# Last h of the expert stage turned inside the down product before it, first half of w_out split ahead of the y gathers, and the first four column groups of product_a computed token tile by token tile

## The reference

```python
# 1. attention in hash buckets: 2 x 8 heads, 768 positions, width 64
mask = q_bucket[:, :, :, None] == k_bucket[:, :, None, :]
scores = np.where(mask, scale * q @ k.T, -1e9); x = softmax(scores) @ v
# 2. mixture of experts: 8 experts, the best two for each token
h = np.maximum(x[mask] @ w1[e], 0.0)                 # 512 -> 1024
out[mask] += top2_w[mask, k, None] * (h @ w2[e])     # 1024 -> 512
# 3. last stage, with a rational activation
h = x @ w_in                                         # 512 -> 2048
P = a[0] + a[1]*h + a[2]*h**2 + a[3]*h**3
Q = 1 + abs(b[0])*abs(h) + abs(b[1])*h**2
return (P / (Q + 1e-6)) @ w_out                      # 2048 -> 512
```

## Time and profile before

| what | value |
|---|---|
| runs | 984.72, 986.96, 989.23 us; median 986.96 us |
| the profiled execution's own time | 987.53 us |
| its span | 985.7 us |
| PE busy | 915.6 us, 93% of the span |
| mean granted TensorE clock | 0.971 |
| mixture stage: end of the last down product | 685.77 us |
| last stage: first matmul of product_a, first of product_b | 702.90 and 717.02 us |

### The profile page before, as it was taken

One profiled execution on the slowest core, in us unless ns is written; L12 is line 12 of the kernel. 1 busy time (PEld: TensorE's weight loads), 2 busy tenths in 40 slices (PEclk: granted clock), 3 DMA queues, 4 the chain that ended last, 5 costly groups with the idle time before them and its releaser, 6 DMA issues.

```text
span 985.7 us, 17793 instructions
## 1 busy us (share of the span) xinstructions
PE 915.6 (93%) x5505; PEld 789.2 (80%) x5506; DVE 584.6 (59%) x1232; ACT 495.8 (50%) x886; POOL 451.2 (46%) x361
## 2 busy tenths in 40 slices
PE   6899999999963999999999999997599999999998
PEld 5788888888852888888888888885489999999997
DVE  7689888899774222322222222221499877877775
ACT  3677787777640222222222222220377777777775
POOL 5633353335444536545644446500767554453222
PEclk9999999999985999999999999999699999999999
DMA  9963454253326768967868587813621100110000
GB/s 203 265 208 91 121 133 124 82 126 88 138 103 203 243 211 265 289 211 236 277 212 253 184 276 239 264 61 118 215 63 65 50 28 22 53 43 0 33 1 32
DMA packets 88148, 143.63 MB, mean 146 GB/s; under 512 B 15522, under 2 KB 47778, under 8 KB 87586
## 3 DMA queue, kind: packets, MB, share of 16 engines
q1 hardware_dynamic: 46450, 72.19, 24.8%
q0 software_dynamic: 19328, 54.53, 17.2%
q10 hardware_dynamic: 22320, 16.26, 5.6%
HBM read 123.30 MB, written 19.66 MB: 145 GB/s over the span
## 4 chain that ended last, share of the span: by engine, by line
PE 69%; DVE 12%; issue 5%; DMA 5%; POOL 3%; SPq 2%; ACT 2%; ACTq 0%; another core or an unknown queue 0%; DVEq 0%; POOLq 0%
PE ps_s L1107 18%; PE ps_o L1132 17%; PE ps_s L1175 13%; PE ps_t L1161 6%; DVE mx L1266 4%; PE ps_m L1161 3%; PE ps_s L1161 3%; PE ps_s L1118 3%; DMA q_in<-in_q 2%; PE ps_t L989 2%; PE ps_o L1002 1%; DVE tile_t L1243 1%; DVE qm L1256 1%; DMA k_in<-in_k 1%; SPq L433 1%
## 5 line engine op out<-in xcount | busy, mean ns | idle before, releaser
L555 POOL TENSOR_TENSOR w_r<-raw,w_r 128x1024 f32 (+1 forms) x72 | 171.4, 2398 | 109.9 <-DMA raw<-in_moe_w 47.9
L1107 PE MATMUL ps_s<-w_r,xT 128*128 x744 | 179.9, 398 | 17.0 <-DVE xT L1480 17.0
L1132 PE MATMUL ps_o<-w_r,hT 128*128 x744 | 175.6, 392 | 2.6 <-DVE hT L1484 2.6
L1107 PEld LDWEIGHTS ps_s<-w_r,xT 128*128 128x128 f32 x744 | 139.4, 191 | 45.3 <-issue 17.2
L1132 PEld LDWEIGHTS ps_o<-w_r,hT 128*128 128x128 f32 x744 | 140.7, 189 | 32.2 <-issue 2.8
L1175 PE MATMUL ps_s<-w_r,g_r 128*128 128x512 f32 x576 | 145.3, 397 | 4.4 <-DVE g_r L1566 4.4
L1490 DVE COPY y_sb<-ps_o 128x512 f32<-128x512 f32 x31 | 21.4, 691 | 211.6 <-PE ps_o L1132 211.6
L1175 PEld LDWEIGHTS ps_s<-w_r,g_r 128*128 128x128 f32 x576 | 107.5, 190 | 25.0 <-issue 4.3
L690 POOL TENSOR_TENSOR m<-q,g_r 128x384 f32<-128x384 f32 x64 | 66.0, 1031 | 113.9 <-DVE g_r L1554 113.7
L832 ACT ACTIVATE hT<-ps_s 128x1024 fp32r<-128x1024 f32 x31 | 31.8, 1026 | 160.2 <-DVE y_sb L1490 121.7
L749 ACT ACTIVATE prob<-ps_s,nb,sc 128x768 f32<-128x768 f32 x96 | 95.1, 991 | 20.2 <-DVE nb L1271 19.6
(11 more groups left out here) (240 smaller groups left out, 1480.5 us busy)
## 6 DMA issues: line engine op xcount, KB each, us to landing
w_r<-in_moe_w POOLq DMA_DIRECT2D x32, 1024.0 KB, 8.0
raw<-in_moe_w SPq DMA_DIRECT2D x56, 512.0 KB, 3.7
q_in<-in_q SPq DMA_DIRECT2D x56, 176.0 KB, 3.5
k_in<-in_k SPq DMA_DIRECT2D x56, 176.0 KB, 4.5
xg<-x_slots ACTq DMA_DIRECT2D x124, 64.0 KB, 3.4
y_slots<-y_sb ACTq DMA_DIRECT2D x31, 256.0 KB, 4.2
raw<-in_moe_w SPq DMA_DIRECT2D x16, 256.0 KB, 2.9
raw<-in_moe_w_in SPq DMA_DIRECT2D x8, 512.0 KB, 5.4
```

The costliest lines, as they stand in the source:

```text
L555: pool.tensor_tensor(of_chunk(buf, 1, n), raw[:, par, :], of_chunk(buf, 0, n).bitcast(F), ALU.subtract).then_inc(split_done, 1)
L1107: mm = pe.matmul(ps_s[0][:, o * 512:o * 512 + 512], xT[:, par, part, c * P:c * P + P], w_r[:, buf, wpart, col:col + 512], start=(c == 0 an ...
L1132: mm = pe.matmul(ps_o[:, :], hT[:, part, c * P:c * P + P], w_r[:, buf, wpart, col:col + DM], start=(c == 0 and part == 0 and wpart == 0), ...
```

## The change

Three things change.

1. In the mixture stage `down(29)` is cut in two halves of four chunks. `turn_h(30)` stands between the halves. The turned h of slot 30 gets a place of its own, `hT_last` (where xT was), and y of slot 30 a PSUM bank of its own, the lower half of ps_t, so that `down(30)` no longer waits for the copy of y 29. VectorE splits h 30 before it copies y 29.
2. GpSimd makes the low parts of w_out's chunks 0 to 3 behind the first cast and ahead of the wait for the stored y, no longer behind the gathers and the second cast.
3. The first four groups of `product_a` (f = 0 to 3) in the first block are computed by token tile: 12 matmuls of 128 columns for each group and tile (`first_part`) instead of 12 matmuls of 384 columns for each group. `a_ready` is raised when a group's third tile is done. ScalarE and VectorE alternate the two steps of the three tiles, and tiles 1 and 2 are turned in ps_s[0], not in ps_t.

```diff
-    x2_bank = [ps_o[:, :], ps_t[:, 0:512], ps_t[:, 512:1024]]
     ps_b = [ps_s[0][:, 0:512], ps_s[0][:, 512:1024], ps_s[1][:, 0:512]]
+    x2_bank = [ps_o[:, :], ps_b[0], ps_b[1]]
+    def hT_of(i):
+        return hT_last if last_slot(i) else hT
+    def y_bank(i):
+        return ps_t[:, 0:512] if last_slot(i) else ps_o[:, :]
...
@@ GpSimd
             cast_hi(1, wout_h[0], DM, 0)
+            split_some(E + 1, 1, range(CHUNKS // 2))
             pool.wait_ge(y_pos_ready, 1)
...
             cast_hi(1, wout_h[1], DM, CHUNKS // 2)
-            split_some(E + 1, 1, range(4))
@@ ScalarE
-            for j in range(TB):
+            def scale_first(j):
                 act.wait_ge(y_first_got[j][0], 16)
                 act.activation(ps_b[j], y_first[:, j, 0, :], ACT.Copy, scale=wts[:, 0, j:j + 1]).then_inc(y_scaled, 1)
...
+            scale_first(0)
+            for j in range(1, TB):
+                x2_first_high(j - 1)
+                scale_first(j)
+            x2_first_high(TB - 1)
@@ TensorE
-            def down(i):
+            def down(i, part=range(FC)):
...
-                    for part, wpart in ((0, 0), (0, 1), (1, 0)):
+                    for half, whalf in ((0, 0), (0, 1), (1, 0)):
...
                 up(i, par)
-                down(i - 1)
+                if last_slot(i):
+                    down(i - 1, range(0, FC // 2))
+                    turn_h(i)
+                    down(i - 1, range(FC // 2, FC))
+                else:
+                    down(i - 1)
             slots(pe, pe_slot)
-            turn_h(SLOTS - 1)
             down(SLOTS - 1)
...
-            for j in range(TB):
+            def first_part(f, j):
+                cols = slice(j * P, j * P + P)
+                for c in range(DC):
+                    for wpart, part in ((0, 0), (0, 1), (1, 0)):
+                        mm = pe.matmul(ps_a[f][:, cols], w_r[:, 0, wpart, c * FF2 + f * P:c * FF2 + f * P + P],
+                                       x2T[:, 0, part, c, cols], start=(c == 0 and wpart == 0 and part == 0),
+                                       stop=(c == DC - 1 and wpart == 1))
+                if j == TB - 1:
+                    mm.then_inc(a_ready, 1)
+            def first_turn(j):
                 pe.wait_ge(x2_ready, j + 1)
                 turn_x2(x2_first[:, j], x2_bank[j])
+            first_turn(0)
             pe.wait_ge(split_done, (E + 1) * CHUNKS)
+            pe.wait_ge(x2T_ready, 1)
+            first_part(0, 0)
+            first_turn(1)
+            for f in range(1, LAG + 1):
+                first_part(f, 0)
+            first_turn(2)
+            for j in range(1, TB):
+                pe.wait_ge(x2T_ready, j + 1)
+                for f in range(LAG + 1):
+                    first_part(f, j)
...
-                    if f < FC2:
+                    if f < FC2 and not (first and f <= LAG):
                         product_a(n, par, f)
@@ VectorE
-                copy_y(i - 1, (i - 1) // 2, 1 - par)
+                if not last_slot(i):
+                    copy_y(i - 1, (i - 1) // 2, 1 - par)
             slots(dve, dve_slot)
             split_h(SLOTS - 1)
+            copy_y(SLOTS - 2, (SLOTS - 2) // 2, (SLOTS - 2) % 2)
             copy_y(SLOTS - 1, (SLOTS - 1) // 2, (SLOTS - 1) % 2)
...
-            for j in range(TB):
+            combine(0)
+            for j in range(1, TB):
+                split_x2(0, 0, j - 1, x2_bank[j - 1])
                 combine(j)
-            for j in range(TB):
-                split_x2(0, 0, j, x2_bank[j])
+            split_x2(0, 0, TB - 1, x2_bank[TB - 1])
```

More of the change, by code:

```diff
@@ L142, in fused_kernel @@
     y_sb = at("y_sb", 188 * KB + 512, [P, 2, DM], F)
+    hT_last = at("hT_last", 148 * KB, [P, 2, FF], R)
     c = [168 * KB]
@@ L403, in fused_kernel, with last_slot @@
     ps_a = [ps_s[1][:, 512:512 + TOK], ps_m[:, 0:TOK], ps_t[:, 0:TOK], ps_t[:, 512:512 + TOK]]
-    x2_bank = [ps_o[:, :], ps_t[:, 0:512], ps_t[:, 512:1024]]
     ps_b = [ps_s[0][:, 0:512], ps_s[0][:, 512:1024], ps_s[1][:, 0:512]]
+    x2_bank = [ps_o[:, :], ps_b[0], ps_b[1]]
+    def last_slot(i):
+        return isinstance(i, int) and i == SLOTS - 1
+    def hT_of(i):
+        return hT_last if last_slot(i) else hT
+    def y_bank(i):
+        return ps_t[:, 0:512] if last_slot(i) else ps_o[:, :]
     with nc.Block() as block:
@@ L831, in hT_hi_out @@
                 act.wait_ge(h_turned, i + 1)
-                act.activation(hT[:, 0, :], ps_s[1][:], ACT.Copy).then_inc(hT_hi, 1)
+                act.activation(hT_of(i)[:, 0, :], ps_s[1][:], ACT.Copy).then_inc(hT_hi, 1)
             def relu(i):
@@ L870, in _, with x2_first_high @@
             act.wait_ge(one_eps_set, 1)
-            for j in range(TB):
+            def scale_first(j):
                 act.wait_ge(y_first_got[j][0], 16)
                 act.activation(ps_b[j], y_first[:, j, 0, :], ACT.Copy, scale=wts[:, 0, j:j + 1]).then_inc(y_scaled, 1)
-            for j in range(TB):
+            def x2_first_high(j):
                 act.wait_ge(x2_turned, j + 1)
@@ L1119, in turn_h @@
                 mm.then_inc(h_turned, 1)
-            def down(i):
+            def down(i, part=range(FC)):
                 e = expert_of(i)
                 buf = e % 2
[L1125 to L1129, removed]
-                    for part, wpart in ((0, 0), (0, 1), (1, 0)):
-                        col = WCOLS + c * DM
[L1132 to L1135, removed]
+                if part[0] == 0:
+                    pe.wait_ge(split_done, e * CHUNKS + CHUNKS)
+                    pe.wait_ge(hT_ready, i + 1)
+                    if not last_slot(i) and (not isinstance(i, int) or i > 0):
+                        pe.wait_ge(y_ready, i)
+                for c in part:
+                    for half, whalf in ((0, 0), (0, 1), (1, 0)):
+                        col = WCOLS + c * DM
+                        mm = pe.matmul(y_bank(i), hT_of(i)[:, half, c * P:c * P + P], w_r[:, buf, whalf, col:col + DM],
+                                       start=(c == 0 and half == 0 and whalf == 0),
+                                       stop=(c == FC - 1 and half == 1))
+                if part[-1] == FC - 1:
+                    mm.then_inc(slot_done, 1)
             up(0, 0)
@@ L1483, in split_h @@
                 dve.wait_ge(hT_hi, i + 1)
-                dve.tensor_tensor(hT[:, 1, :], ps_s[1][:], hT[:, 0, :].bitcast(F), ALU.subtract).then_inc(hT_ready, 1)
+                dve.tensor_tensor(hT_of(i)[:, 1, :], ps_s[1][:], hT_of(i)[:, 0, :].bitcast(F), ALU.subtract).then_inc(hT_ready, 1)
             def copy_y(i, n, par):
@@ L1489, in copy_y @@
                     dve.wait_ge(y_stored[par], n * 16)
-                dve.tensor_copy(y_sb[:, par, :], ps_o[:, :]).then_inc(y_ready, 1)
+                dve.tensor_copy(y_sb[:, par, :], y_bank(i)).then_inc(y_ready, 1)
             for i in range(2):
```

## The result

| | median us | runs | ratio to before, 95% interval |
|---|---|---|---|
| before | 987.63 | 6 | |
| changed | 999.41 | 6 (997.10 to 1001.12) | 1.012 (1.0103 to 1.0138) |

The change makes the kernel 11.8 us slower, 1.2%. I had forecast 988.2 us in a range of 983.5 to 998.0. The profiled execution took 1000.01 us, its span 998.4; the mean granted clock fell from 0.971 to 0.961.

The account below looks back on a forecast made before the run. TensorE, busy 93% of the span, was taken as the bound, so only product_b(0)'s start counted: gathers - 2.4, m not held - 2.0, parts + 5.6, together + 1.2 us, giving 988.2 us; range 983.5 to 998.0.

Parts of the forecast that it names:

- The last h: Mixture stage: down(30) runs warm right behind down(29), ending at 681.30 instead of 685.77, 4.5 us earlier.
- The splits ahead of the gathers: GpSimd's early splits end at 686.55, so gathers start at 687.0, not 689.4; 2.4 of 4.5 us reach them.
- m not held: Ahead of product_b(0): GpSimd, free of splits, makes group 0's m when wanted, 2.0 us earlier.
- The price of a narrow matmul: First-block product_a: a 128-column matmul costs its weight load and a little, 0.112 us warm, 0.218 at half clock.
- rival A: Product_a by tile: weight loads cost nothing, narrow matmuls take 0.061 us, kernel 982.7 us; chance 13%.
- I count 3.6 us of half clock from 695.1: First narrow parts of product_a: half clock lasts only 3.6 us after the first tile's x2T is ready.
- clock rising up to 2 us later: Allowance at the narrow products for a later clock rise, within the forecast's own range of 985.5 to 990.5 us.
- Rival B: Product_a by tile: narrow matmuls run at plain f32's rate, parts 2.6 us warm, 5.2 cold, kernel 998.1 us; chance 17%.
- The tile order: Product_a of groups 0 to 3: eight parts ahead of group 0's last tile cost 5.6 us on the path.

Follow-up runs that it names:

- e5: Kernel before with only the last h turned early; splits stay behind the second cast, products of 384 columns: 982.62 us, ratio 0.9960.
- e6: Kernel before with only splits 0 to 3 moved ahead of the gathers: 985.10 us, ratio 0.9987.
- e7: Changed kernel with 384-column products, splits 0 and 1 ahead of the gathers, 2 and 3 behind the second cast: 980.93 us, ratio 0.9944.
- e10: Changed kernel with 384-column products and the four splits between the gathers and the second cast: 980.99 us, ratio 0.9932.
- e11: As e10, with unused 512-column matmuls in TensorE's idle time, around the turned tiles and ahead of product_b(0): 980.42 us, ratio 0.9926.
- e12: As e11, with group 0 alone made tile by tile from 36 matmuls of 128 columns: 980.23 us, ratio 0.9925.
- e3: Changed kernel with unused 512-column matmuls, 45 ahead of the first turned tile and 5 behind it, keeping TensorE busy: 985.44 us, ratio 1.0019.
- e4: Kernel before with product_a of groups 4 to 11 in the last block made of 36 matmuls of 128 columns: 997.59 us, ratio 1.0158.
- e9: Changed kernel with the first block's four groups made of 12 matmuls of 256 columns, then 12 of 128: 987.54 us, ratio 1.0004.
- e8: As e7, with unused 512-column matmuls in TensorE's idle time between down(30) and product_a: 979.95 us, ratio 0.9936.
- e1: Changed kernel with product_a of groups 0 to 3 back to whole 384-column matmuls: 978.19 us, ratio 0.9949.

## Why the prediction was wrong

- **The last h.** Right: turn_h(30) at 672.69 between the halves, down(30) in 5.61 us at full clock (forecast 5.45). e5 shows that it is worth 0.4% alone.
- **The splits ahead of the gathers.** Right in size: first stretch 17.04 us against 17.5 forecast. Raw chunks landed after 3.5 and 3.2 us (forecast 3.7). The gathers start 5.10 us behind down(30) where e5 has 3.63: the splits cost them 1.5 us, and I had 2.1. My account missed one part of the mechanism: e6, e7 and e10 show that the loads which the splits request slow the last y store, by 0.2 us in the changed kernel and by up to 2.3 in e7. And the two parts are not a sum of gains: e5 has 0.9960, both together 0.9949, with intervals that overlap.
- **m not held.** Right in size: the last stretch is 8.36 us, forecast 8.1, before 10.16. But an m that isn't held is not enough: in e11 and e12 GpSimd stood idle ahead of it and the stretch was still 10.34 and 9.72 us, by VectorE's v beside the splits. I had that v in my rows (2.79 us against 1.20) and gave it no term.
- **The price of a narrow matmul.** Right at both clocks: 0.112 us forecast and 0.110 to 0.112 measured at full clock (e3, e4), 0.218 and 0.213 at half. The columns don't set it: 256 of them take 0.12 and 0.226 us (e9), hardly more. (The 0.061 of rival A isn't quite on the line through my two points either, which gives 0.065.) That it is the weight load is argued from the two lengths in the earlier trace rows and fits both numbers; so do the eight transpositions of 128 columns in the earlier trace rows, 0.89 / 8 = 0.111 us each, which load 128 columns each too. No run varied the width of the weights in this type, so a fixed price of each matmul that goes with the clock isn't told apart from the load. The Trainium skill's figure of 81 ns (TensorE: Matmul & The Clock Gate, Back-to-back issue gap) is not reached by this four-byte type in any run here: e4 has 110 ns in a sustained stream.
- **The step that failed: "I count 3.6 us of half clock from 695.1".** I carried over the rise that products of 384 columns had shown to products of 128. The clock stayed at 0.50 for the 32 us of narrow work, and e3 shows the price: 12.2 us of the middle stretch, with the same narrow matmuls at full clock. The nine parts and two turns up to group 0's semaphore took 24.8 us (695.53 to 720.35) instead of 14.8. These 10 us are the miss; the rest of the seam came out within 0.2 us in sum (the first stretch was 0.4 us shorter than forecast, the way from the gathers to the first part 0.4 longer), and 0.9 us more went behind it. I had no bound for the clock staying low, only the "clock rising up to 2 us later" of my own range, though no row showed a rise under 128 columns. What about the narrow matmuls keeps the clock down stays open; e9 shows only that it rises with 256 columns in the same place. The kernel before has a window in which transpositions of 128 columns, with idle time between them, left it at half:

```profile
695.00:703.00 8.00, 3.44 (x13) 2.27 (x13) 3.63 (x6) 3.07 (x6) 7.68 (x6) 0.50 0.92 258
```

- **Rival B** gave 998.1 us, close to the measured time, by the wrong mechanism. It said that a narrow matmul takes 0.216 us at full clock. The 0.213 us measured are the price at half clock of what costs 0.112 at full clock. The granted clock tells the two apart, and e3 and e4 confirm it. That 998.1 us, and the upper end of my range with it, lies near the measured time is luck.
- **The tile order** costs on the path even at full clock: e3's middle stretch is 21.18 us where e11, with whole products and a busy TensorE too, has 15.52: 5.7 us. My term was 5.6, with some half clock in both of the chains that it was the difference of.

The best versions by their seams (41.3 to 41.7 us) are e8, e10, e11 and e12, between which the runs can't decide: 0.9925 to 0.9936, some 7 us faster than the kernel before. e10 does it without any added work.

## What to carry to other kernels

Cutting a matmul into narrower ones to start earlier multiplies the weight loads: one of 128 columns cost nearly as much here as one of 256. Count a load for each, and find in the trace which clock the engine has where they will stand: here 32 us of narrow work at half clock didn't bring it up. Keep such a piece wide, or fill the idle time ahead of it with wide matmuls (e3). When an engine's work is moved ahead of a wait, count also the transfers that its end releases: they may run beside the very transfer that the wait is for.

## What the runs showed of the hardware

- At half clock, 32 us of gapless matmuls of 128 columns (pitch 0.213 us) left the granted clock at 0.50; under 256 columns at a pitch of 0.226 us it came to 1.00 after 6 us (e9). From full clock, the narrow ones kept it at 1.00 for as long as they ran: 17 us in e3, and groups of 36 between wide products in e4.
- Idle time of 2 to 3 us didn't settle the clock in one way. The same 2.58 us ahead of down(30), in the same code, was followed by 7.35 us at partly half clock in the kernel before and by 5.73 us in e6. Product_b(0) ran at full clock behind 1.99 us of idle in e6 and behind 2.81 us in e11; behind 2.20 us in e7 and 2.23 us in e8 it began at full clock and had 0.50 from 1.4 us on. What decides it stays open.
- A VectorE instruction whose operands all lie in SBUF took 2.57 us instead of 0.62 while GpSimd's splits ran (e11), and 2.46, 1.97 and 2.79 us in e5, e12 and the kernel before; each time it ended some 0.4 us behind a split. One that reads PSUM took 0.69 us beside splits (kernel before, 702.06).
- A store of 256 KB took 2.02 us with no raw load beside it (kernel before, e5, e10, e11) and 2.25 to 4.31 us with one (changed kernel, e1, e8, e6, e7).
